# A two-product MLP behind windowed attention: TensorE's matmuls recast as pairs of 64-row halves

## The reference, cut to what matters

```python
# x: [4, 4096, 192], weight_gen: [4, 4096, 8, 7]
w = softmax(weight_gen, axis=-1)                     # over the 7 taps
out = np.einsum('bshk,bskhg->bshg', w, x_unfolded)   # 7 shifted copies of x
x = out.reshape(16384, 192)
h = x @ w_in                                         # w_in:  [192, 2048]
relu6 = np.clip(h + 3.0, 0.0, 6.0)
g = h * relu6 / 6.0
return (g @ w_out).astype(np.float32)                # w_out: [2048, 192]
```

## Time and profile before

| what | value |
|---|---|
| median of 3 runs | 1226.31 us (1226.02 to 1226.93) |
| span of the profiled execution, from its first instruction to its last | 1224.4 us |
| TensorE busy | 1194.6 us, 98% |
| VectorE, ScalarE, GpSimd busy | 66%, 52%, 56% |
| mean granted clock of TensorE | 0.999 of 2.4 GHz |
| mean HBM rate | 34 GB/s |

### The profile page before, as it was taken

One profiled execution on the slowest core, in us unless ns is written; L12 is line 12 of the kernel. 1 busy time (PEld: TensorE's weight loads), 2 busy tenths in 40 slices (PEclk: granted clock), 3 DMA queues, 4 the chain that ended last, 5 costly groups with the idle time before them and its releaser, 6 DMA issues.

```text
span 1224.4 us, 19650 instructions
## 1 busy us (share of the span) xinstructions
PE 1194.6 (98%) x6848; PEld 1083.3 (88%) x6848; DVE 803.7 (66%) x1362; ACT 634.2 (52%) x1269; POOL 690.8 (56%) x455
## 2 busy tenths in 40 slices
PE   1999999999999999999999999999999999999998
PEld 1899999999999999999999999999999999998997
DVE  7866657576665766656666575766657666566665
ACT  3455555455555555545555554555555555455554
POOL 7893854909358192762918549094581927729100
PEclk9999999999999999999999999999999999999999
DMA  6101010010101001010010100101010010100000
GB/s 179 46 22 58 20 45 13 20 58 20 58 0 65 14 20 58 0 65 13 20 58 20 45 13 20 58 20 58 0 56 22 20 58 0 65 13 13 13 14 13
DMA packets 12071, 42.08 MB, mean 34 GB/s; under 512 B 1183, under 2 KB 5279, under 8 KB 10139
## 3 DMA queue, kind: packets, MB, share of 16 engines
q1 hardware_dynamic: 12059, 41.93, 9.8%
HBM read 29.34 MB, written 12.58 MB: 34 GB/s over the span
## 4 chain that ended last, share of the span: by engine, by line
PE 96%; DVE 1%; POOL 1%; issue 0%; DMA 0%; ACT 0%; DVEq 0%; ACTq 0%
PE work L464 48%; PE sums L482 32%; PE sums L484 15%; PE work L444 2%; POOL pool_acc L154 0%; POOL pool_prod L152 0%; DVE w_in L404 0%; DMA w_raw<-weight_gen_dram 0%; DVE work L350 0%; DVE w_out L410 0%; DVE g_lo L361 0%; DVE out_stage L381 0%; POOL pool_acc L147 0%; POOL pool_prod L148 0%; DVE xt_b L373 0%
## 5 line engine op out<-in xcount | busy, mean ns | idle before, releaser
L350 DVE SCALAR_TENSOR_TENSOR work<-relu,work 128x512 f32<-128x512 f32 x512 | 355.2, 694 | 402.9 <-ACT relu L254 402.8
L482 PE MATMUL sums<-w_out,g_hi 128*128 128x384 f32 x2048 | 614.1, 356 | 0.7 <-DVE g_lo L361 0.7
L254 ACT ACTIVATE relu<-work 128x512 f32<-128x512 f32 x512 | 306.4, 598 | 554.0 <-PE work L464 549.3
L484 PE MATMUL sums<-w_out,g_lo 128*128 128x192 f32 x2048 | 513.0, 251 | 0.0
L464 PE MATMUL work<-xt_a,w_in 128*128 128x512 f32 x1536 | 449.3, 400 | 2.0 <-DVE xt_b L373 2.0
L482 PEld LDWEIGHTS sums<-w_out,g_hi 128*128 128x128 f32 x2048 | 384.3, 188 | 23.7 <-DVE g_lo L361 1.3
L484 PEld LDWEIGHTS sums<-w_out,g_lo 128*128 128x128 f32 x2048 | 389.8, 190 | 15.8
L361 DVE TENSOR_TENSOR g_lo<-work,g_hi 128x512 fp32r<-128x512 f32 x512 | 349.7, 683 | 2.1
L464 PE MATMUL work<-xt_b,w_in 128*128 128x512 f32 x1024 | 318.1, 392 | 0.0
L264 ACT CAST g_hi<-work 128x512 fp32r<-128x512 f32 x512 | 299.3, 585 | 11.4 <-DVE work L350 11.3
L147 POOL TENSOR_TENSOR pool_acc<-x_in,w_soft 128x768 f32<-128x768 f32 (+1 forms) x32 | 50.0, 1563 | 442.7 <-DVE w_soft L341 429.7
(11 more groups left out here) (31 smaller groups left out, 203.7 us busy)
## 6 DMA issues: line engine op xcount, KB each, us to landing
x_in<-x_dram SPq DMA_DIRECT2D x15, 1344.0 KB, 6.0
out_dram<-out_stage SPq DMA_DIRECT2D x32, 384.0 KB, 2.8
w_raw<-weight_gen_dram SPq DMA_DIRECT2D x16, 224.0 KB, 3.0
w_out_raw<-moe_w_out_dram SPq DMA_DIRECT2D x1, 1152.0 KB, 13.5
x_in<-x_dram SPq DMA_DIRECT2D x1, 768.0 KB, 5.1
w_in_raw<-moe_w_in_dram SPq DMA_DIRECT2D x1, 768.0 KB, 8.9
w_in_raw<-moe_w_in_dram SPq DMA_DIRECT2D x2, 384.0 KB, 10.3
w_out_raw<-moe_w_out_dram SPq DMA_DIRECT2D x1, 384.0 KB, 6.6
```

The lines of the kernel that those rows point to most:

```text
L254: nc.scalar.activation(t.relu[:, m % 2, :], t.work[m % BANKS][:], ACT.Relu, bias=3.0).then_inc(s.relu_ready, 1)
L350: nc.vector.scalar_tensor_tensor(bank[:], t.relu[:, m % 2, :], 6.0, bank[:], ALU.min, ALU.mult).then_inc(s.gated, 1)
L482: nc.tensor.matmul(t.sums[n][:, 0:2 * D], t.g_hi[:, m % BANKS, cols], t.w_out[:, j, :], start=(j == 0), stop=False)
L484: ins = nc.tensor.matmul(t.sums[n][:, D:2 * D], t.g_lo[:, m % BANKS, cols], t.w_out[:, j, 0:D], start=False, stop=(j == TILES - 1))
```

## The change

The rows of TensorE's array are split in two halves for all matmuls: rows 0 to 63 ("upper" in the code) and rows 64 to 127 ("lower"). Each matmul with K = 128 becomes two with K = 64 and the same number of columns, one for each half, and these are issued alternately so that the two halves work on two different banks. Slots are taken in pairs ("duos"): `fill_first` has the upper half work for the first tile of the duo and the lower half for the second, `fill_second` swaps them. The fifth matmul is issued for 256 columns only, since each half now takes only the tokens whose hi rows lie in it (`block_b`).

In the second product, `multiply` goes through the four `sums` in two groups of two banks: part 0 with one assignment of halves to banks, part 1 with the other. Part 1's start on a group waits until part 0's last matmul on that group is finished (`multiplied_first`); `fill_second` waits likewise for `filled_first`. The transposes are split in the same way.

TensorE's order becomes, for duo d: `fill_first(d)`, `multiply(2d-3)`, `fill_second(d)`, `multiply(2d-2)`; around the transposes `multiply` of slot 11 is parted over two duos. ACT does two `relu`s and then two `g_hi`s, DVE two `gate`s and then two `g_lo`s, and both put the evacuation of `sums` ahead of the duo after the first one of a new group. `g_hi` and `g_lo` have six buffers in place of four.

```diff
+G_SLOTS = 6
+DUOS = ROUND // 2
+HALF_DUOS = SLOTS // 2
+TRANSPOSE_DUO = GROUP_SLOTS.index(TA) // 2
+SHIFT_AT, EXP_AT, SUM_AT, SCALE_AT = 2, 2, 3, 4
+ROWS = [slice(0, DB), slice(DB, P)]
...
 def scalar_program(nc, act, dram, t, s):
...
+    def duo(q, d, last=False):
+        if d == HALF_DUOS + 1:
             evacuate(q, 0)
+        if d == DUOS + 1:
             evacuate(q, 1)
...
+        if is_tile(2 * d):
+            relu(q, 2 * d)
+            relu(q, 2 * d + 1)
+            g_hi(q, 2 * d)
+            g_hi(q, 2 * d + 1)
...
 def vector_program(nc, dve, t, s):
...
+        if is_tile(2 * d):
+            gate(q, 2 * d)
+            gate(q, 2 * d + 1)
+            g_lo(q, 2 * d)
+            g_lo(q, 2 * d + 1)
...
 def tensor_program(nc, pe, t, s):
...
+    def products(m, r):
+        half, j = slot(m)
+        bank = t.work[m % BANKS]
+        rows = ROWS[r]
+        cols = slice(j * P, (j + 1) * P)
+        hi_b = bank.rearrange("p (i o c) -> p i o c", o=2, c=P)[:, :, r, :]
+        return [(bank[:], t.w_in[rows, 0, 0, cols], t.xt_a[rows, half, 0, :]),
+                (bank[:], t.w_in[rows, 0, 0, cols], t.xt_a[rows, half, 1, :]),
+                (bank[:], t.w_in[rows, 1, 0, cols], t.xt_a[rows, half, 0, :]),
+                (bank[:], t.w_in[rows, 0, 1, cols], t.xt_b[rows, half, :]),
+                (hi_b, t.w_in[rows, 1, 1, cols], block_b(t, half, r, r))]
...
+    def fill_first(q, d, last=False):
...
+        for i, (upper, lower) in enumerate(zip(products(2 * d, 0), products(2 * d + 1, 1))):
+            nc.tensor.matmul(*upper, start=(i == 0), stop=False)
+            ins = nc.tensor.matmul(*lower, start=(i == 0), stop=False)
+        ins.then_inc(s.filled_first, 1)
+
+    def fill_second(q, d, last=False):
...
+        pe.wait_ge(s.filled_first, duos_filled(q, d))
+        both = list(zip(products(2 * d + 1, 0), products(2 * d, 1)))
+        for i, (upper, lower) in enumerate(both):
+            ins_upper = nc.tensor.matmul(*upper, start=False, stop=(i == len(both) - 1))
+            ins_lower = nc.tensor.matmul(*lower, start=False, stop=(i == len(both) - 1))
...
         pe.wait_ge(s.g_lo_ready, tiles_done(q, m))
+        for part in parts:
+            turn = (part + j) % 2
+            for group in range(2):
+                sets = (2 * group, 2 * group + 1)
+                if part == 1:
+                    pe.wait_ge(s.multiplied_first, 2 * tiles_done(q, m) - 1 + group)
+                for n in sets:
+                    rows = ROWS[(n + 1 + turn) % 2]
+                    if j == 0 and not first and part == 0:
+                        pe.wait_ge(s.out_staged, GT * 2 * q + GT * (m // SLOTS - 1) + n + 1)
+                    nc.tensor.matmul(t.sums[n][:, 0:2 * D], t.g_hi[rows, m % G_SLOTS, n * P:(n + 1) * P],
+                                     t.w_out[rows, j, :], start=(j == 0 and part == 0), stop=False)
+                for n in sets:
+                    rows = ROWS[(n + 1 + turn) % 2]
+                    ins = nc.tensor.matmul(t.sums[n][:, D:2 * D], t.g_lo[rows, m % G_SLOTS, n * P:(n + 1) * P],
+                                           t.w_out[rows, j, 0:D], start=False,
+                                           stop=(j == TILES - 1 and part == 1))
+                    if j == TILES - 1 and part == 1:
+                        ins.then_inc(s.sums_ready, 1)
+                if part == 0:
+                    ins.then_inc(s.multiplied_first, 1)
+
+    def duo(q, d, last=False):
+        h = d % HALF_DUOS
+        bank_free(q, 2 * d - 3, last)
+        fill_first(q, d, last)
+        if h == TRANSPOSE_DUO + 1:
+            multiply(q, 2 * d - 3, (0,), last)
+        elif h == TRANSPOSE_DUO + 2:
+            multiply(q, 2 * d - 5, (1,), last)
+            multiply(q, 2 * d - 3, (0, 1), last)
+        else:
+            multiply(q, 2 * d - 3, (0, 1), last)
+        fill_second(q, d, last)
+        multiply(q, 2 * d - 2, (0, 1), last)
```

More of the change, by code:

```diff
@@ L80, in tiles_done, with duos_filled, transposes_done @@
     return 2 * TILES * q + sum(is_tile(i) for i in range(m + 1))
[L83 to L85 removed]
+def duos_filled(q, d):
+    return tiles_done(q, 2 * d + 1) // 2
+def transposes_done(q, d):
+    return 1 + 2 * q + sum(i % HALF_DUOS == TRANSPOSE_DUO for i in range(d + 1))
 def inputs_split(q, m):
@@ L351, in gate, with g_lo @@
                                        ALU.min, ALU.mult).then_inc(s.gated, 1)
[L353 to L365, removed]
+    def g_lo(q, m):
+        dve.wait_ge(s.g_hi_ready, tiles_done(q, m))
+        nc.vector.tensor_tensor(t.g_lo[:, m % G_SLOTS, :], t.work[m % BANKS][:], f32(t.g_hi[:, m % G_SLOTS, :]),
+                                ALU.subtract).then_inc(s.g_lo_ready, 1)
     def x_lo(half, what, bank):
@@ L438, in tensor_program, with transposes @@
 def tensor_program(nc, pe, t, s):
-    def transpose_set(half, what, bank):
+    def transposes(half, what, bank, r):
         src = t.attn_a if what == TA else t.attn_b
[L443 to L447, removed]
+        rows = ROWS[r]
+        return [(bank[:, i * P + r * DB:i * P + (r + 1) * DB], src[rows, half, i * P:(i + 1) * P], t.ident[rows, rows])
+                for i in range(GT if what == TA else GT // 2)]
@@ L449, in fill, with bank_free @@
+    def bank_free(q, m, last=False):
         if skipped(m, last):
             return
[L451 to L456, removed]
-            return
[L458 to L467, removed]
+        if is_tile(m):
+            pe.wait_ge(s.g_lo_ready, tiles_done(q, m))
+        else:
+            pe.wait_ge(s.xt_lo_ready, inputs_split(q, m))
+    def fill_first(q, d, last=False):
+        if skipped(2 * d, last):
+            return
+        if not is_tile(2 * d):
+            pe.wait_ge(s.attn_ready, 4 * q + 2 * (d // HALF_DUOS) + 2)
+            pe.sem_inc(s.attn_taken, 1)
+            transpose_first(1 - slot(2 * d)[0], t.work[2 * d % BANKS], t.work[(2 * d + 1) % BANKS])
+            return
+        for i, (upper, lower) in enumerate(zip(products(2 * d, 0), products(2 * d + 1, 1))):
+            nc.tensor.matmul(*upper, start=(i == 0), stop=False)
+            ins = nc.tensor.matmul(*lower, start=(i == 0), stop=False)
+        ins.then_inc(s.filled_first, 1)
@@ L469, in multiply @@
+    def multiply(q, m, parts, last=False, first=False):
         if skipped(m, last):
             return
-        half, j = slot(m)
+        j = slot(m)[1]
         if not is_tile(m):
@@ L499, in tensor_program @@
     pe.wait_ge(s.w_in_lo, 2)
-    for m in range(1, EARLY):
-        fill(0, m + AHEAD)
-        multiply(0, m)
+    duo(0, FIRST_DUO)
     pe.wait_ge(s.w_out_lo, 2)
     with pe.Fori(0, PAIRS - 1) as q:
[L506 to L511, removed]
+        for d in range(FIRST_DUO + 1, FIRST_DUO + 1 + DUOS):
+            duo(q, d)
@@ L514 @@
+    for d in range(FIRST_DUO + 1, DUOS):
+        duo(PAIRS - 1, d, last=True)
+    for m in range(ROUND - 3, ROUND):
+        multiply(PAIRS - 1, m, (0, 1), last=True)
 class Semaphores:
```

163 lines of the change are left out of this document (91 added, 72 removed).

## The result

| | before | after |
|---|---|---|
| median | 1226.26 us | 1272.87 us (4 runs, 1270.32 to 1281.89) |
| ratio after / before | | 1.039, 95% interval 1.0368 to 1.0412 |
| profiled execution | span 1224.4 us | 1273.59 us, span 1271.5 us |
| mean granted clock of TensorE | 0.999 | 0.983 |

The kernel is 3.9% slower. The forecast was 1209 us and faster.

A forecast was written before the change was run, and what follows sets the result against it. TensorE, busy for 98% of the span, was taken as the bound. 1224.4 - 55 + 10 + 12 + 15 + 1 = 1207.4 us, with the median 1.9 us above the span: 1209 us, range 1180 to 1300.

The forecast's parts named there:

- Columns saved: First product: the fifth pass goes from 512 to 256 columns, saving 0.107 us a tile, -55 us.
- Rivals 3: Weight loads of both halves share one path, 0.107 us a load, lengthening the second product: about 1540 us, chance 0.12.
- rival 4: Issue of 26 matmuls a tile in place of 13 sets a floor on TensorE: 1266 to 1300 us, chance 0.09.
- 5: Rival: the 0.02 us in each matmul step that is not streaming overlaps between halves: 1140 to 1180 us, chance 0.06.
- 6: Rival: the halves take turns in place of overlapping, 2.18 us more a tile: about 2300 us, chance 0.03.
- The wait inside `multiply`: Second product: part 1 waits for part 0's last matmul on its banks, 0.02 us late once a tile, +10 us.
- Behind the transposes: Ahead of slot 14, TensorE waits on the other engines' chain, 0.38 us with restart in 32 groups, +12 us.
- Evacuation: At a new group TensorE reaches the fourth `sums` bank before DVE frees it: 0.49 us with restart, 31 times, +15 us.
- Transposes 0: Six transposes a group become eight half steps with half the columns: -7 to +7 us, taken as 0.
- start and end +1 us: A second gate before the first `g_lo` and the last two `sums` together: +1 us, between -3 and +4.
- The rest: Remaining effects: transposes 0, start and end +1 us; ACT and DVE order, softmax parts, buffers and GpSimd cost nothing.
- rival 2: Halves overlap, but each new wait costs its full restart or the two stalls double: 1226 to 1266 us, chance 0.12.

The follow-up runs named there:

- e6: e1 with the fifth pass put back to 512 columns in each half: 1261.18 us, ratio 1.0283 against the kernel before.
- e1: The in-line version: the changed kernel with TensorE's loop over 15 rounds written out, same matmuls and waits: 1215.11 us, ratio 0.991 against the kernel before.
- e8: The kernel before with only the fifth pass in halves of 256 columns, all other matmuls full: 1390.13 us, ratio 1.134.
- e3: The kernel before with three rounds in TensorE's loop body and five turns, full matmuls only: 1230.23 us, ratio 1.0032.
- e10: e3 with one more wait ahead of the branch, of TensorE on its own last matmul: 1250.33 us, ratio 1.0197 against the kernel before.
- e9: The changed kernel with TensorE's loop branch moved behind fill_first, same instructions in the same order: 1261.72 us, ratio 1.0288 against the kernel before.

## Why the prediction was wrong, point by point

- **Columns saved, -55 us: right.** 0.11 us a tile; run e6 shows 46 us, which is the saving less the cover that the longer pass gives to the late places. Rivals 3 (one path for the loads), 4 (issue), 5 and 6 are out: loads stand in pairs, starts of two halves 0.01 us apart, `multiply` at 1.15 us with 16 matmuls, two at a time.
- **The wait inside `multiply`, +10 us: right**, 0.03 us a tile, 15 us. Its price uncovered was right as well. What I did not see is its second effect, below.
- **Behind the transposes, +12 us: right.** `fill_second(8)` takes 1.38 us in place of 1.06, and the next `multiply` 0.10 more: 0.42 x 32 = 13 us.
- **Evacuation, +15 us: half.** 0.22 us in place of 0.49, 7 us. The sum took four times the mean record of 0.348 us for DVE's four operations, 1.39 us. But their records overlap, and four in a row take 1.15 (before the change too, 1.14), so the last bank is free 0.24 us sooner. From e1:

```profile
514.33 1.15 DVE L360 SCALAR_TENSOR_TENSOR out_stage<-sums,out_stage 128x192 f32<-128x192 f32 x4
```

- **Transposes 0, start and end +1 us: a little short.** With the two `multiply`s among them the transposes of a group take 3.08 us in e1 (534.17 to 537.25) and took 2.89 before (500.85 to 503.74); less 0.03 for the wait inside each `multiply`, that is 0.13 us a group, 4 us. The first transposes of the loop come at 57.07 us in e1, 54.31 before: 2.8 us. All these terms as measured give about 1210 of the 1213.3 us of the in-line version; 3 us are not assigned.
- **"The rest" is the step that failed.** Against the forecast span of 1207.4 us the in-line version has 1213.3, and the changed kernel 1271.5. The 58 us between the last two are the loop's branch, which stands in no term of the sum. I doubled the matmuls in a written-out body and asked of that only whether they could be issued fast enough (rival 4), not where the instructions come from. The trace of the kernel before had the sign of it, 7 instruction packets in the whole run and none between 111 and 1169 us: the body was fetched once and stayed.
- **The waits' price.** I priced each wait of TensorE on itself by the time that it adds when nothing else goes wrong. Such a wait also keeps the sequencer from running ahead. With it the queue held 0.2 us of work at the branch, without it 2.7. So a stop that costs the kernel before 1.1 us costs the changed one 3.2 and mostly a fall of the clock, 1.6 more.

The range (1180 to 1300) held the time, and the direction was wrong: the 2.5 us bound of "faster" was missed by 49 us, and rival 2's 1226 to 1266 and rival 4's 1266 to 1300 named other causes. That 1272.87 lies inside the range, and in rival 4's part of it, is luck. The prediction's own test of its mechanism, a duo of 4.3 to 4.5 us, came out as forecast while the time went the other way, since it looked only at the steady state. Its signs of the two late places, 32 and 31 idle rows, don't show in the list of waits: TensorE's records overlap, so a delay of 0.31 us from start to start leaves 0.14 us of idle time (337.83 to 337.97), and it must be read from the starts.

**Still open.** That the stop is a fetch is read from the packets beside it and from the effect of the body's length; nothing shows the fetch itself ending it. How long a body may be: on TensorE's rows a turn has 907 instructions in the kernel before and 973 in e8, and both stay; 1800 in the changed kernel, which stayed in two turns of 14 (899 and 973 us) for a reason that no run shows; and 2715 in e3, which never stayed. A loop over one group in place of a round, which would halve the body, wasn't tried. Why the clock falls behind some stops of the same length and not behind others is open too, and so is the one run of the changed kernel that took 1281.89 us, of which there is no trace.

## What to carry to other kernels

Where a change multiplies the instructions of a written-out loop body, look at the instruction queue and at the loop's branch in the trace: if the body stays loaded, ask whether it still will. Here the same body in straight line had its fetches and no wait. A wait of an engine on itself costs its own time and also the run-ahead, which in the kernel before hid 2.7 of a 3.7 us stop; so put the branch where much is queued, and cover such waits well. Array halves paid here only through the columns that went away, and only with every matmul in halves; one change to halves and back in each tile cost more than it saved. And a wait that the list puts down to an engine long done is to be looked up on the sequencer's own rows.

## What the runs showed of the hardware that I had not expected

- The branch back on TensorE stands for 3.3 to 3.9 us with packets of the instruction queue beside it, in bodies of 1800 instructions and more, and for 0.21 us without them.
- Behind idle times of TensorE of 3.0 to 3.5 us its clock fell to 1.2 GHz in 11 of 12 cases (the changed kernel), behind 3.6 to 4.1 us in 4 of 4 (e10), behind 2.1 to 2.7 us in 7 of 14 (e9), and behind 0.5 to 1.1 us in none of 4 (e3). The fall came within 1.7 us after matmuls ran again, in one case 0.25 us ahead of that (432.60 against 432.85), and cost about 1.6 us.
- Two halves of 64 rows stream and load weights side by side, in steps as long as those of full rows (starts within 0.00 to 0.04 us of each other), and going from full rows to halves and back costs about 0.37 us (e8).
